# Attention with four load buffers, keys stored once, and the mix weights converted between the tiles

## What is computed

```python
# 1. attention in chunks of 32 queries: each sees 8 memory keys and the keys
#    from 16 before its chunk to 8 behind it (56), 64 in all
scores = scale * np.matmul(q_c, concat([mem_k, k_ctx]).T)
a = np.exp(scores - max(scores)); a = a / (sum(a) + 1e-09)
out[:, :, c_start:c_end] = np.matmul(a, concat([mem_v, v_ctx]))
# 2. channel mix, with each token and the one before it
xk = mu_k * x + (1 - mu_k) * x_prev;  xr = mu_r * x + (1 - mu_r) * x_prev
k = np.maximum(xk @ w_k, 0);  x = sigmoid(xr @ w_r) * (k * k @ w_v)
# 3. a mixture of 8 experts; a gate picks one for each token (or keeps the
#    expert of the token before), h = relu(x @ w1[e]), out = p[e] * (h @ w2[e])
```

## Time and profile before

| | |
|---|---|
| median of 3 runs | 531.59 us (530.92 to 531.82) |
| profiled execution | 533.26 us, span 531.5 us, mean granted TensorE clock 0.919 |
| busy share of the span | TensorE 83%, weight loads 69%, VectorE 46%, ScalarE 40%, GpSimd 10% |
| HBM read, written | 55.41 MB, 12.62 MB |

### The profile page before, as it was taken

One profiled execution on the slowest core, in us unless ns is written; L12 is line 12 of the kernel. 1 busy time (PEld: TensorE's weight loads), 2 busy tenths in 40 slices (PEclk: granted clock), 3 DMA queues, 4 the chain that ended last, 5 costly groups with the idle time before them and its releaser, 6 DMA issues.

```text
span 531.5 us, 10141 instructions
## 1 busy us (share of the span) xinstructions
PE 440.0 (83%) x3759; PEld 366.4 (69%) x3759; DVE 245.9 (46%) x477; ACT 212.7 (40%) x319; POOL 55.3 (10%) x62
## 2 busy tenths in 40 slices
PE   1667628999999999999940069999999999999993
PEld 1545518889898989989830047777777777777772
DVE  2454575653535234354045149222382247464861
ACT  1333474663435253344022038222462245555750
POOL 0000000010100101010003601111111111111110
PEclk9967867999999999999975569999999999999998
DMA  8668442428000000000004779511173128383810
GB/s 302 253 208 294 157 181 86 152 90 309 0 0 0 0 0 0 0 0 1 2 0 158 238 281 406 209 54 40 52 227 136 40 71 253 141 251 132 271 61 10
DMA packets 18313, 67.31 MB, mean 127 GB/s; under 512 B 2734, under 2 KB 2734, under 8 KB 18288
## 3 DMA queue, kind: packets, MB, share of 16 engines
q1 hardware_dynamic: 13104, 50.92, 27.9%
q0 software_dynamic: 4896, 16.05, 8.8%
q10 hardware_dynamic: 288, 0.02, 0.0%
HBM read 55.41 MB, written 12.62 MB: 128 GB/s over the span
## 4 chain that ended last, share of the span: by engine, by line
PE 67%; DMA 14%; issue 7%; DVE 5%; POOL 3%; ACT 2%; SPq 1%; POOLq 0%; DVEq 0%; ACTq 0%
PE PS L530 16%; PE PS L403 12%; PE PS L513 12%; PE PS L435 10%; DMA QK<-tiles 5%; PE PS L419 5%; DMA XR<-grouped_rows 5%; POOL grouped_rows L1107 2%; PE PS L521 2%; PE PS L453 2%; PE PS L504 1%; PE PS L330 1%; PE PS L357 1%; DMA RAW<-wmix 1%; PE PS L343 1%
## 5 line engine op out<-in xcount | busy, mean ns | idle before, releaser
L1022 DVE TENSOR_TENSOR ELO<-ERAW,EHI 128x1024 fp32r<-128x1024 f32 x56 | 66.8, 1219 | 12.9 <-ACT EHI L696 10.3
L696 ACT ACTIVATE EHI<-ERAW 128x1024 fp32r<-128x1024 f32 x56 | 57.4, 1053 | 29.6 <-DMA ERAW<-wexp 20.8
L403 PE MATMUL PS<-XHI,WHI 128*128 128x256 f32 x192 | 56.6, 295 | 1.2 <-DVE WLO L805 1.2
L530 PE MATMUL PS<-EHI,HH 128*128 128x512 f32 x128 | 54.6, 426 | 2.6 <-issue 1.0
L403 PE MATMUL PS<-XHI,WLO 128*128 128x256 f32 x192 | 55.2, 287 | 0.0
L403 PE MATMUL PS<-XLO,WHI 128*128 128x256 f32 x192 | 55.1, 287 | 0.0
L513 PE MATMUL PS<-EHI,XSH 128*128 128x512 f32 x128 | 53.0, 414 | 1.4 <-DVE XSL L1030 1.4
L1043 DVE TENSOR_TENSOR HL<-PS,HH 128x512 fp32r<-128x512 f32 x32 | 22.1, 691 | 66.3 <-ACT HH L716 65.9
L513 PE MATMUL PS<-ELO,XSH 128*128 128x512 f32 x128 | 51.5, 402 | 0.0
L513 PE MATMUL PS<-EHI,XSL 128*128 128x512 f32 x128 | 51.2, 400 | 0.0
L530 PE MATMUL PS<-EHI,HL 128*128 128x512 f32 x128 | 50.6, 395 | 0.0
(11 more groups left out here) (141 smaller groups left out, 774.6 us busy)
## 6 DMA issues: line engine op xcount, KB each, us to landing
ERAW<-wexp SPq DMA_DIRECT2D x56, 512.0 KB, 5.6
QK<-tiles SPq DMA_DIRECT2D x12, 768.0 KB, 5.7
VV<-tiles SPq DMA_DIRECT2D x12, 520.0 KB, 3.9
grouped_rows<-ZR POOLq DMA_DIRECT2D x1, 5140.0 KB, 18.1
RAW<-wmix SPq DMA_DIRECT2D x10, 512.0 KB, 3.8
XR<-grouped_rows POOLq DMA_DIRECT2D x17, 257.0 KB, 4.2
CO<-consts SPq DMA_DIRECT2D x1, 470.0 KB, 6.5
rows_out<-OSB,OIDX POOLq DMA_INDIRECT x16, 3.9
```

Source lines behind the costliest of these rows:

```text
L403: last = nc.tensor.matmul(PS[q % 2][:, half * 256:half * 256 + 256], w[:, c:c + P], x[:, k, :], start=n == 0, stop=n == 11)
L530: last = nc.tensor.matmul(PS[4][:, :], x[:, f, :], ww[:, c:c + D], start=n == 0, stop=n == 23)
L696: nc.scalar.activation(EHI[w][:, c * CH2:(c + 1) * CH2], ERAW[c][:], ACT.Copy).then_inc(ehi_done, 1)
L1022: nc.vector.tensor_tensor(ELO[w][:, c * CH2:(c + 1) * CH2], ERAW[c][:], EHI[w][:, c * CH2:(c + 1) * CH2].bitcast(F32), ALU.subtract).then_ ...
```

## The change

The key part of a tile's load now holds each key of the tile's window once (KWIN = 152 keys for each head pair), and the memory keys stand behind it once for each head pair. So scores() does, for each head pair, two matmuls of 128 queries with the 8 memory keys, and then the eight matmuls of 32 queries as before, but with 56 keys each. QK and VV have four buffers, RAW three. The attention loop is written out for all 12 tiles. The RAW loads are issued between the tile loads, and weight_hi(t-2) and weight_lo(t-2) run at the end of step t; mix_scaled and mix_full for the first pair run at t = 6 and 7, mix_hi and mix_lo at t = 8 and 9. The first load of constants brings the identity alone; the tables come behind all others, and who needs them waits for tables_in. The waits for V and QK moved from probs_transposed() to values() and scores(). The values' layout is unchanged.

```diff
-QW, KW, VWT = HP * P, HP * CPT * KEYS, HP * CPT * VW
-INW = QW + KW + VWT
+KWIN = LEFT + P + RIGHT
+QW, KW, MW, VWT = HP * P, HP * KWIN, HP * NMEM, HP * CPT * VW
+QKW = QW + KW + MW
+INW = QKW + VWT
...
+NBUF = 4
+NRAW1 = 3
...
+            def raw_load(n):
+                if n >= NRAW1:
+                    sp.wait_ge(wlo_done, n - NRAW1 + 1)
+                sp.dma_start(RAW[n % NRAW1][:], wmix[:, n * CH1:(n + 1) * CH1]
+                             ).then_inc(raw_loaded[n % NRAW1], 16)
+
+            qk_load(0)
+            sp.dma_start(CO[:, 0:C_LT], consts[:, 0:C_LT]).then_inc(const_in, 16)
+            qk_load(1)
+            v_load(0)
+            v_load(1)
+            for t in range(2, NBUF):
+                qk_load(t)
+                v_load(t)
+            for t in range(NBUF, NT):
+                sp.wait_ge(scores_done, t - NBUF + 1)
+                qk_load(t)
+                sp.wait_ge(pv_done, t - NBUF + 1)
+                v_load(t)
+                raw_load(t - NBUF)
+            for n in range(NT - NBUF, N1):
+                raw_load(n)
+            sp.dma_start(CO[:, C_LT:CW], consts[:, C_LT:CW]).then_inc(tables_in, 16)
...
                 for hp in range(HP):
+                    for par in range(2):
+                        r = slice(DH * par, DH * par + DH)
+                        o = hp * KEYS
+                        nc.tensor.matmul(PS[2 * u + par][:, o:o + NMEM], q[r, hp, :], m[r, hp, :],
+                                         start=True, stop=True)
                     for par in range(2):
                         r = slice(DH * par, DH * par + DH)
                         for c in range(CPT):
                             last = nc.tensor.matmul(
-                                PS[2 * u + par][CHUNK * c:CHUNK * (c + 1), hp * KEYS:(hp + 1) * KEYS],
-                                q[r, hp, c * CHUNK:(c + 1) * CHUNK], k[r, hp, c, :], start=True, stop=True)
+                                PS[2 * u + par][CHUNK * c:CHUNK * (c + 1), o + NMEM:o + KEYS],
+                                q[r, hp, c * CHUNK:(c + 1) * CHUNK],
+                                k[r, hp, c * CHUNK:c * CHUNK + KEYS - NMEM], start=True, stop=True)
...
+            def attention(t):
+                u = t % 2
+                probs_out(t, u, t < 2)
+                if t:
+                    x_out(t - 1)
+                if t + 2 < NT:
+                    exps(t + 2, u, False)
+                if t >= 2:
+                    weight_hi(t - 2)
+                if t in (6, 7):
+                    mix_scaled(0, t - 6, True)
+                if t in (8, 9):
+                    mix_hi(0, t - 8, True)
...
+            def attention(t):
+                u = t % 2
+                if t + 2 < NT:
+                    shifted(t + 2, u, False)
+                normed(t, u, t < 2)
+                if t >= 2:
+                    weight_lo(t - 2)
+                if t in (6, 7):
+                    mix_full(0, t - 6, True)
+                if t in (8, 9):
+                    mix_lo(0, t - 8, True)
...
                 squared(g, 2, first)
                 if first:
-                    weight_lo(N1A + 2)
+                    dve.wait_ge(tables_in, 16)
+                    nc.vector.tensor_copy(X2R[:, :, D + 1], CO[:, C_TOK:C_TOK + NT])
```

More of the change, by code:

```diff
@@ L94, in moe_program @@
         assert top[0] <= after_rows
+        top[0] = work
+        QK = [place(f"QK{i}", [P, QKW]) for i in range(2, NBUF)]
+        VV = [place(f"VV{i}", [P, VWT]) for i in range(2, NBUF)]
+        RAW = [place(f"RAW{i}", [P, CH1]) for i in range(2, NRAW1)]
+        assert top[0] <= after_rows
         top[0] = after_rows
@@ L244, in _ @@
         def _(sp):
[L245 to L281, removed]
+            def qk_load(t):
+                sp.dma_start(QK[t % NBUF][:], tiles[t, :, 0:QKW]).then_inc(qk_loaded[t % NBUF], 16)
+            def v_load(t):
+                sp.dma_start(VV[t % NBUF][:], tiles[t, :, QKW:INW]).then_inc(v_loaded[t % NBUF], 16)
@@ L345, in probs_transposed, with values @@
                 last.then_inc(pt_done, 1)
[L347 to L348 removed]
+            def values(t):
+                u = t % 2
+                pe.wait_ge(v_loaded[t % NBUF], 16 * (t // NBUF) + 16)
                 pe.wait_ge(pt_evac, t + 1)
[L350 removed]
+                if t:
                     pe.wait_ge(norm_done, t)
[L352 removed]
+                v = VV[t % NBUF][:].rearrange("p (h c n) -> p h c n", h=HP, c=CPT)
                 for hp in range(HP):
@@ L361, in values, with x_transposed @@
                 last.then_inc(pv_done, 1)
-            def x_transposed(t, u, first):
+            def x_transposed(t):
                 pe.wait_ge(norm_done, t + 1)
-                if not first:
+                if t:
                     pe.wait_ge(xt_evac, t)
@@ L368, in x_transposed @@
                     last = nc.tensor.transpose(PS[7][:, k * P:(k + 1) * P],
-                                               XN[u][:, k * P:(k + 1) * P], ident)
+                                               XN[t % 2][:, k * P:(k + 1) * P], ident)
                 last.then_inc(xt_done, 1)
[L372 to L385, removed]
+            scores(0)
+            scores(1)
+            for t in range(NT):
+                probs_transposed(t)
+                if t + 2 < NT:
+                    scores(t + 2)
+                if t:
+                    x_transposed(t - 1)
+                values(t)
+            x_transposed(NT - 1)
             pe.wait_ge(wlo_done, N1A)
@@ L586, in weight_hi @@
             def weight_hi(n):
-                act.wait_ge(raw_loaded[n % 2], 16 * (n // 2 + 1))
-                nc.scalar.activation(WHI[:, n * CH1:(n + 1) * CH1], RAW[n % 2][:],
+                act.wait_ge(raw_loaded[n % NRAW1], 16 * (n // NRAW1 + 1))
+                nc.scalar.activation(WHI[:, n * CH1:(n + 1) * CH1], RAW[n % NRAW1][:],
                                      ACT.Copy).then_inc(whi_done, 1)
[L591 to L606, removed]
+            def attention(t):
+                u = t % 2
+                probs_out(t, u, t < 2)
+                if t:
+                    x_out(t - 1)
[7 more added lines that the diff above has]
+                    mix_hi(0, t - 8, True)
             def mix_scaled(g, kind, first):
@@ L633, in _ @@
             exps(1, 1, True)
-            over_pairs(act, attention)
+            for t in range(NT):
+                attention(t)
             x_out(NT - 1)
@@ L849, in _ @@
             shifted(1, 1, True)
-            over_pairs(dve, attention)
+            for t in range(NT):
+                attention(t)
             dve.sem_inc(logit_evac, 1)
@@ L886, in mix @@
                     logits_out(2 * g - 1)
-                else:
-                    weight_lo(N1A + 1)
                 squared(g, 2, first)
                 if first:
-                    weight_lo(N1A + 2)
+                    dve.wait_ge(tables_in, 16)
+                    nc.vector.tensor_copy(X2R[:, :, D + 1], CO[:, C_TOK:C_TOK + NT])
                 squared(g, 3, first)
-                if first:
-                    for n in range(N1A + 3, N1):
-                        weight_lo(n)
                 if not last:
```

74 lines of the change are left out of this document (27 added, 47 removed).

## The result

| | before | after |
|---|---|---|
| median, runs on the same chip | 531.71 us (530.92 to 533.51) | 540.9 us (538.36 to 542.35) |
| ratio, 95% interval | | 1.0165 [1.0126, 1.0204] |
| profiled execution | 533.26 us, span 531.5 | 542.35 us, span 540.6 |

The prediction was 521.7 us with a range up to 530, and it was wrong in sign. First the windows of the stages in the changed kernel; the borders are the first transposes, the start of step 10, the start of up(), and the starts of the second and the third mix iteration (columns as in the earlier trace rows).

A forecast was written before the change was run, and what follows sets the result against it. Late QK loads left no attention engine full; afterwards TensorE would bind. up() at 73.7 instead of 82.9 gives -9.2, the first mix iteration 0.7, together -9.9: 533.26 - 9.9 - 1.67 = 521.7 us, range 513 to 530.

The forecast's parts named there:

- The QK wait goes.: Attention: with four buffers the waits for QK loads (17.8 us at L343) vanish; TensorE itself may be late next.
- Scores of 2.6 us at full clock, 1.8 to 3.7.: Attention, TensorE: a tile's rewritten scores take 2.6 us at full clock, between 1.8 and 3.7; before 0.79.
- A step of 4.6 fast, about 7 slow.: Attention: TensorE's work for one tile step takes 4.6 us at full clock, 7 us at the low one.
- The mean step I take as 5.0: ... one step in seven or so low.: Attention: steps average 5.0 us, mixing 4.6 at full clock with 7 at the low one; steps 0 to 9 take 50.0.
- The second rival: Attention: scores cost more than loads saved, as tile changes drain TensorE and its clock stays low; kernel 543 us; chance 12%.
- Writing the loop out adds code to fetch ... I take 0.: Attention loop: fetching the added straight code costs 0 us, judged by the first pair and the fast step behind it.
- VectorE's 1.5 us.: Attention: mix work moved onto VectorE, in steps t = 6 to 9, is charged 1.5 us in all.
- Start at 14.0.: Attention start: the first transposes begin at 14.0 us (14.8 before), with gate weights holding the constants until 6.8.
- Tail and mix.: Attention's end: step 10 takes 2.9 us, tail 5.9; first mix iteration gives back 0.7 us of idle, near 31.1.
- All later starts 10 us earlier, same durations.: Behind the first mix iteration: everything starts 10 us earlier and lasts as long as before.

The follow-up runs named there:

- wide_first_two_ahead: change_two_ahead with all eight wide memory matmuls of a tile issued ahead of its 64 narrow ones: 534.28 us, ratio 1.0053.
- filled kernels: The change, and change_two_ahead, each with eight bf16 matmuls of unread output added to each tile: 539.33 us and 538.12 us.
- old_keys_new_schedule: The change with the key layout and scores of before, keeping four buffers, written-out loop and moved weight work: 527.49 us, ratio 0.9921.
- old_keys_two_ahead: The change with keys and scores of before, two buffers, TensorE's loop over two tiles, QK loads issued ahead: 526.28 us, ratio 0.9924.
- change_filled: The change with eight bf16 matmuls (128x128 weights by 256 columns, output unread) added to each tile: 539.33 us, ratio 1.0166.
- written_out_only: The kernel before, with only the attention loops of TensorE, ScalarE and VectorE written out for all tile pairs: 537.39 us, ratio 1.0092.
- change_two_ahead: The change with two buffers, TensorE's loop over two tiles and QK loads issued ahead, keeping its keys and scores: 542.12 us, ratio 1.0187.

## Why the prediction was wrong, step by step

- **"The QK wait goes."** Right: no wait of L350 for DMA is left of the 17.8 us. TensorE itself was late next, as said.
- **Scores of 2.6 us at full clock, 1.8 to 3.7.** A little high: 2.32. Per entry I had taken 0.17 us from the earlier trace rows, measured are 0.09 fast and 0.12 slow; the wide matmuls took 0.99 where 0.8 to 1.6 was forecast. The rule of the Trainium skill (TensorEngine Tiling (Array Packing), "Key Properties"), that a change of the tiling mode drains TensorE, agrees with the runs: wide_first_two_ahead took six changes out of each tile and 7.8 us out of the kernel.
- **A step of 4.6 fast, about 7 slow.** Right: 4.75 and 6.79.
- **"The mean step I take as 5.0: ... one step in seven or so low."** This is the step that failed. From the first transposes to those of step 10 went 68.08 us, 6.8 a step, where 50.0 - 0.6 + 1.5 = 50.9 were forecast: 17.2 us more. Only 2 of 24 groups of transposes were at the full clock. I argued from the mix stage, always busy and at full clock, and from the slow stretch with waits in each step, and took it that filling the waits would raise the clock. The filled kernels show TensorE at 97% busy with a granted clock of 0.50 and at 95% busy with 0.93, so being busy is not enough. Before, 12 of 24 groups were short; half of the steps, not one in seven, was the row to start from. Even the half would not have done: with my 4.6 and 7 us it gives a mean step of 5.8, up() at 81.7 and 529.7 us, still faster than before. The loss needs the low clock in nearly all steps. The second rival was the case, with 12% of my chances, and its working ended near the truth (a mean step of 7.15, up() at 95.2 and 543 us; measured 6.81, 91.67 and 540.9), but by luck: it took scores of 3.7 us at the full clock, which were 2.32, and the low clock in only half of the steps.
- **"Writing the loop out adds code to fetch ... I take 0."** Wrong too. In the kernel before it costs 5.9 us, in the old keys' schedule up to 3.84 us a stall. In the change itself 3.8 us of stalls show inside groups. I had judged by the first pair and the fast step behind it, which shows no wait for code, and one step does not speak for twelve. The profile of before has 15 instruction packets, the change's has 23; the range had no term for them.
- **VectorE's 1.5 us.** Not seen as a charge: no wait for VectorE or ScalarE above 0.2 us stands in the ten steps; with TensorE slower than foreseen, they had room.
- **Start at 14.0.** It was 12.86: the constants were waited for until 5.42, not 6.8, as the gate weights landed in 3.6 us instead of 5.5.
- **Tail and mix.** From step 10 to up() 10.73 us instead of 2.9 + 5.9 = 8.8, at a clock of 0.50; VectorE's waits are the same as before (2.0 for L376 and L368). The first mix iteration was 30.60, predicted 31.1.
- **"All later starts 10 us earlier, same durations."** Nearly: 418.3 against 416.8 us; I did not trace these 1.5 us.

Put in numbers, in the profiled execution's time: forecast 533.26 - 9.9 = 523.4; 17.2 more for the ten steps, of which 3.8 are stalls inside groups (1.47 + 0.84 + 1.49); 1.9 for step 10 and the tail; 1.1 less at the start, 0.5 less in the first mix iteration; 1.5 behind it. That makes 542.4, and 542.35 was measured.

**Where the expected gain went.** Without the new keys the rest of the change brought 4.0 us (old_keys_new_schedule, 527.49 against 531.52 in that batch), and 4.1 in a loop (old_keys_two_ahead, 526.28 against 530.38), where some 10 were expected of the whole. In the first, waits for code took the place of those for QK; in the second, 12.5 us of waits for QK were left, with two buffers. A version that has neither wait, four buffers and a short loop, was tried once (528.42), and there ScalarE and VectorE are late. I found no version measurably better than 526.3; the intervals of 0.9921 and 0.9924 can't be told apart.

**What stays open.** What makes the clock rise was not isolated: the added matmuls bring wider outputs, more 128-row tiles and another type at once. How much of change_filled's time is the fill's own, how much a clock that it bought, is known only from the steps. Why the code comes late is open too. That its packets stand behind loads in the DMA engines would fit the stall of 3.84 us in old_keys_new_schedule (94% DMA share from 26 to 32 us). It does not fit the change itself, whose stall of 1.47 us came while the DMA engines moved nothing:

```profile
32.10:33.50 1.40, 0.00 (x1) 0.00 (x0) 0.00 (x0) 1.10 (x2) 0.00 (x0) 1.00 0.00 0
```

The code packet next to it moved before it, between 31.25 and 31.5 us. In the stall of 1.49 us the DMA share is 0.02 (65.50 to 66.97), and in that of 2.36 us of written_out_only 0.04 (66.10 to 68.39). The runs show that straight code has such stalls and that a loop which has run once has none; they do not show what the engine waits for in them.

## What to carry to other kernels

Before bytes are traded for matmuls, cost these at the clock that the stage really has, by counting its short and long groups, with the low clock throughout as one end of the range, and not at the clock that it would have if it were busy: here small matmuls kept TensorE busy for 97% of a stretch at 0.50. Keep matmuls of one tile size together; splitting them into groups cost 0.09 to 0.12 us for each change of size, here 7 to 8 us of 542. And give the code that a written-out loop adds a term of its own, here 5.9 us: a stall called "issue" in the middle of a group, at a place that drifts from tile to tile, is its sign.

## What the runs showed of the hardware that I had not expected

- A 64-row tile of 128 queries by 8 keys is not cheap for its 8 columns: 0.11 us each at the low clock and 0.06 at the full one (0.99 by 16), while the 32-wide ones of 56 keys start every 0.016 and 0.012 us (1.03 and 0.77 by 64).
- A TensorE that has no gap at all can be granted 0.50 of its clock for over 20 us (57 to 81 us of change_two_ahead), and the same program with more work in it 0.93.
- Stalls inside groups, of up to 3.84 us, came with straight code and not in a loop's second turn, although a code packet is only 16 KB; some came with full DMA queues (0.96 from 27.70 to 31.50 us of old_keys_new_schedule) and some with empty ones.
